# The order of SyncE's first loads and stores, and of GpSimd's first five steps, in a fused attention and two-layer kernel

## The reference

```python
q_d = q.reshape(B, H, Sd, 4, D).mean(axis=3)         # k_d, v_d likewise; Sd = 144
out_up = np.repeat(sm_attn(q_d, k_d, v_d), 4, axis=2)   # attention over pooled positions
mask = np.abs(pos[:, None] - pos[None, :]) < 4          # each position sees 7 neighbours
out_local = softmax(where(mask, scale * q @ k.T, -1e9)) @ v
x = (out_up + out_local)    # as 2304 tokens x 512
x = ((x @ w_a) * (x @ w_b)) @ w_out                     # 512 -> 1536 -> 512
h = x @ w_in                                            # 512 -> 1024
solu = h * softmax(h)
out = layernorm(solu) * g_ln @ w_out2                   # 1024 -> 512
```

## Time and profile before

| what | value |
|---|---|
| median of 3 runs | 793.23 us (791.5 to 793.58) |
| profiled execution, its own time | 793.58 us |
| its span, first to last instruction | 791.4 us |
| TensorE busy | 759.7 us, 96% of the span |
| TensorE busy from 0 to 160 us | 133.3 us |
| VectorE busy | 560.9 us, 71% |
| ScalarE, GpSimd busy | 298.2 us (38%), 214.7 us (27%) |
| DMA | 117.27 MB, 148 GB/s in the mean |
| TensorE's granted clock, mean | 0.998 of full speed |

### The profile page before, as it was taken

One profiled execution on the slowest core, in us unless ns is written; L12 is line 12 of the kernel. 1 busy time (PEld: TensorE's weight loads), 2 busy tenths in 40 slices (PEclk: granted clock), 3 DMA queues, 4 the chain that ended last, 5 costly groups with the idle time before them and its releaser, 6 DMA issues.

```text
span 791.4 us, 12269 instructions
## 1 busy us (share of the span) xinstructions
PE 759.7 (96%) x4440; PEld 695.3 (88%) x4440; DVE 560.9 (71%) x975; ACT 298.2 (38%) x819; POOL 214.7 (27%) x260
## 2 busy tenths in 40 slices
PE   6878889899999999999999999999999999999998
PEld 5767888799999999999999999999988888888886
DVE  4579999979979787778777876022467666666663
ACT  3443655454353525344524424224322212222222
POOL 2467977638414421041001111121100000000000
PEclk9999999999999999999999999999999999999999
DMA  9999958584887586683956433637121011011011
GB/s 189 192 237 221 217 117 258 199 259 149 265 244 243 169 244 183 186 203 106 256 163 188 149 107 110 205 102 228 39 66 54 27 54 54 27 55 53 27 41 41
DMA packets 96652, 117.27 MB, mean 148 GB/s; under 512 B 19921, under 2 KB 59603, under 8 KB 96593
## 3 DMA queue, kind: packets, MB, share of 16 engines
q1 hardware_dynamic: 81872, 106.98, 49.0%
q10 hardware_dynamic: 14721, 9.51, 4.2%
HBM read 95.62 MB, written 20.84 MB: 147 GB/s over the span
## 4 chain that ended last, share of the span: by engine, by line
PE 79%; DVE 0%; ACT 0%; issue 0%; DVEq 0%
PE psum L851 25%; PE psum L853 24%; PE psum L852 24%; PE psum L963 2%; PE psum L807 1%; PE psum L787 1%; PE psum L797 1%; PE psum L818 1%; PE psum L769 0%; DVE acc L1470 0%; DVE accT L1479 0%; ACT p_pool L1059 0%; ACT out_sb L1262 0%; ACT out_d L1077 0%; DVE ab_f L1381 0%
## 5 line engine op out<-in xcount | busy, mean ns | idle before, releaser
L851 PE MATMUL psum<-x_hi,w_hi 128*128 128x384 f32 x576 | 199.5, 346 | 2.3 <-DVE x_lo L1375 1.4
L853 PE MATMUL psum<-x_hi,w_lo 128*128 128x384 f32 x576 | 194.1, 337 | 0.0
L852 PE MATMUL psum<-x_lo,w_hi 128*128 128x384 f32 x576 | 193.9, 337 | 0.0
L851 PEld LDWEIGHTS psum<-x_hi,w_hi 128*128 128x128 f32 x576 | 109.2, 190 | 6.5 <-issue 4.6
L852 PEld LDWEIGHTS psum<-x_lo,w_hi 128*128 128x128 f32 x576 | 109.4, 190 | 0.0
L853 PEld LDWEIGHTS psum<-x_hi,w_lo 128*128 128x128 f32 x576 | 109.0, 189 | 0.0
L1381 DVE TENSOR_TENSOR ab_f<-psum,a_sb 128x384 f32<-128x384 f32 x72 | 39.8, 553 | 90.9 <-PE psum L853 62.0
L851 PE MATMUL psum<-ab_hi,wo_hi 128*128 128x384 f32 x288 | 99.8, 346 | 3.3 <-issue 3.3
L853 PE MATMUL psum<-ab_hi,wo_lo 128*128 128x384 f32 x288 | 96.6, 335 | 0.0
L852 PE MATMUL psum<-ab_lo,wo_hi 128*128 128x384 f32 x288 | 96.4, 335 | 0.0
L1689 POOL TENSOR_TENSOR raw<-raw 96x256 f32<-96x256 f32 x60 | 55.5, 951 | 123.2 <-DMA raw<-in_q 59.2
(11 more groups left out here) (147 smaller groups left out, 1420.0 us busy)
## 6 DMA issues: line engine op xcount, KB each, us to landing
wo_hi<-wo_hi_scratch SPq DMA_DIRECT2D x53, 256.0 KB, 2.7
wo_lo<-wo_lo_scratch SPq DMA_DIRECT2D x53, 256.0 KB, 3.1
k_u<-in_k SPq DMA_DIRECT2D x11, 576.0 KB
v_u<-in_v SPq DMA_DIRECT2D x11, 576.0 KB
k_u<-in_k SPq DMA_DIRECT2D x17, 288.0 KB
v_u<-in_v SPq DMA_DIRECT2D x17, 288.0 KB
wo_raw<-in_moe_w_out SPq DMA_DIRECT2D x19, 256.0 KB, 4.9
raw<-in_v SPq DMA_DIRECT2D x8, 576.0 KB, 6.7
```

Of the source, the lines that this page charges most:

```text
L851: mm(dst, wh, xh, start=first, stop=False, skip_group_check=not check)
L852: mm(dst, wh, xl, start=False, stop=False, skip_group_check=not check)
L853: last = mm(dst, wl, xh, start=False, stop=end, skip_group_check=not check)
```

## The change

Three things change. In SyncE's list for the head, the first block of w_out and the two stores of pooled v of batch 0 go ahead of the unit loads of q and k; the loads of w_out's second block and of weights 1 go ahead of raw (1, 2); the third block of w_out goes ahead of raw (1, 0); and the two stores of batch 1 go ahead of the wait for `x_summed` and of `load_weights(2)`. On GpSimd, `normalise(2)` goes between the two halves of the sums of pooled v. The two waits ahead of GpSimd's later sums are written as one expression: for tau 0 it still wants `x_lo_ready` at PPB = 4, and for tau 2 it now wants `hp_normed` at 4 where it wanted 2.

```diff
             load_weights(0)
+            load_wo(0)
+            store_vd(0, 0)
+            store_vd(0, 1)
             load_unit_q(1, 0)
             load_unit_k(1, 0)
-            store_vd(0, 0)
-            store_vd(0, 1)
             load_vd(0)
+            load_wo(1)
+            load_weights(1)
             load_raw(1, 2, 0)
             load_raw(1, 2, 1)
-            load_wo(0)
-            load_wo(1)
-            load_weights(1)
+            load_wo(2)
             load_raw(1, 0, 0)
             load_raw(1, 0, 1)
-            load_wo(2)
+            store_vd(1, 0)
+            store_vd(1, 1)
 
             sp.wait_ge(s.x_summed, PPB)
             load_weights(2)
-            store_vd(1, 0)
-            store_vd(1, 1)
...
             normalise(1)
             pool_rows(0, 2, 0)
+            normalise(2)
             pool_rows(0, 2, 1)
-            normalise(2)
             normalise(3)
             for tau in (2, 0):
 
-                if tau == 2:
-                    pool.wait_ge(s.hp_normed, 2)
-                else:
-                    pool.wait_ge(s.x_lo_ready, PPB)
+                pool.wait_ge(s.hp_normed if tau == 2 else s.x_lo_ready, PPB)
                 for half in range(2):
                     pool_rows(1, tau, half)
```

## The result

The changed kernel is slower: 800.35 us (median of 4 runs, 798.28 to 801.35) against 792.37 us for the kernel before (790.88 to 793.58), a ratio of 1.0098 [1.0069, 1.0127]. That is 8.0 us, four times the forecast of 2.0, and outside the range of 791 to 799.5 us. The execution that was profiled took 798.9 us with a span of 797.1, against 793.58 and 791.4: 5.3 and 5.7 us more.

What follows compares the result with a forecast made beforehand. It took TensorE, 96% of the span, as the bound, with v_d on the path at the head. Between +1.3 (GpSimd's burst) and +2.6 (v_d) it took +2.0: 793.58 + 2.0 = 795.6 us, median 795.5, range 791 to 799.5.

Steps and rivals of the forecast that it cites:

- the relief: Head: raw (1, 2) sums no longer overlap VectorE's last head steps, giving back 1.25 us, bounds 0 and 1.5.
- the lean to slower: Whole kernel: chance 0.45 that it measures slower, against 0.42 same and 0.13 faster.
- When v_d lands: Head: v_d, queued behind the unit loads, first used at 44.3 and not 41.72, so +2.6 us.
- The bytes are the same, and the hole in the DMA is only moved (32 to 35): DMA in the head: same traffic, its idle gap merely shifted to 32 to 35 us, at no cost.
- The rest at nothing: Other loads and stores SyncE issues in a different place or time: their readers have cover, so 0 us.
- Stores (1) land by 63: SyncE: batch 1's stores land by 63 us, so raw (1, 1) goes out near 65 as before.
- GpSimd's burst: First tile: sums from 52.0 to 66.7, then weight_low and wo_low to 71.6, setting the second gate, +1.3 us.
- The burst runs contended: Rival, GpSimd in the first tile: sums at contended lengths, +5.0 us, 798.5 us in all; chance 0.27.
- +1.3 here: First tile: end of GpSimd's sums and low parts at 71.6, 1.3 us later; lower end for the +2.0 taken.
- +2.6 of v_d: Head: lateness of v_d's first use without any relief; upper end for the +2.0 taken.
- everything that it loses is paid: Head: v_d is on the path with 1.77 us of wait, so any delay of it lengthens the kernel.
- the wait itself costs nothing: GpSimd: hp_normed at 4 is met by 51.35, before raw (1, 2) lands at 52, so 0 us.

Runs made afterwards that it cites:

- e3: Changed kernel with load_vd(0) moved ahead of the unit loads of q and k: 799.98 us, ratio 1.0079.
- e12: Kernel before with only load_wo(3) moved, to behind the first load_unit_v: 798.7 us, ratio 1.0072.
- e4: Changed kernel with the two stores of batch 1 back behind load_weights(2): 799.9 us, ratio 1.0083.
- e13: Changed kernel with load_vd(0) ahead of the unit loads, ten of twelve raw (1, 0) additions left out, load_wo(3) ahead of raw (1, 1): 797.66 us, 1.0044.
- e6: Changed kernel with ten of GpSimd's twelve additions for raw (1, 0) left out: 799.82 us, ratio 1.0083.
- e10: Changed kernel with load_wo(3) ahead of the loads of raw (1, 1), nothing left out: 801.33 us, ratio 1.0093.
- e7: Kernel before with ten of GpSimd's twelve additions for raw (1, 0) left out: 793.66 us, ratio 1.0009.
- e8: Kernel before with stores of batch 0, v_d, raw (1, 2) and raw (1, 0) issued ahead of unit loads, wo(1), weights(1): 794.0 us, 1.0019.
- e16: Kernel before with only load_wo(0) and the two stores of batch 0 ahead of the unit loads: 794.98 us, ratio 1.0015.
- e9: Changed kernel with ten of twelve raw (1, 0) additions left out and load_wo(3) ahead of raw (1, 1): 798.38 us, ratio 1.0059.
- e11: e8 with load_wo(3) ahead of raw (1, 1): 792.4 us, ratio 0.9986.
- e14: e11 with the unit load of v moved from n = 3 to n = 6: 793.52 us, ratio 1.0008.
- e15: Kernel before with load_wo(3) ahead of raw (1, 1) and the unit load of v at n = 6: 795.1 us, ratio 1.0022.
- e1: Kernel before with only GpSimd's part of the change: 795.6 us, ratio 1.0024.
- e2: Kernel before with only SyncE's part of the change: 797.35 us, ratio 1.0047.
- e5: Changed kernel with load_raw(1, 2) ahead of load_wo(1) and load_weights(1): 800.47 us, ratio 1.0102.

## Why the prediction was wrong

Right were the first steps on GpSimd and SyncE: `normalise(2)` at 28.70 (about 29 predicted), second sums to 33.0 (33.6), the unit loads at 33.40, `load_vd(0)` at 38.77 (39.2). Right was the relief: v_d is 4.9 us later and the first up product 3.6, so 1.3 us came back, as worked out; with GpSimd idle, `hp_den` took 0.16 us for both pairs and the normalisation 0.45. Right was that all of it lies before 160 us, and the lean to slower (0.45).

1. **"When v_d lands" was mis-sized.** I took 5.1 us from issue to use (39.2 to 44.3), bounds 43.3 to 46; it took 7.8 (38.77 to 46.60). I had let the unit loads run at 220 GB/s from 35.0, but the queue was empty when SyncE began to issue them, and the DMA share was 0.57 from 34 to 38 us, at 151 to 154 GB/s. The four loads of q alone carry 0.38 MB and took 2.65 us to issue, which is 148 GB/s. That v_d stands behind the unit loads is borne out: ahead of them, in e3, it took 4.9 us from issue to use (36.30 to 41.15). The 0.3 to 0.7 us that I allowed from the last byte to the waiting engine stand in no row; block 3 before landed at 78.17 and was read at 78.20. First product: +3.6, not +1.35.

2. **"The bytes are the same, and the hole in the DMA is only moved (32 to 35)" was false in its second half.** The bytes are the same (117.27 MB), but 6.3 us of DMA time are free around it instead of 2.3, and there is a second hole, 60 to 70 us, with 4.9 us. I had drawn the store's wait as a delay for v_d alone. It is one for everything behind it in SyncE's list, and the queue had been nearly full.

3. **"The rest at nothing" failed.** It said that weights(2) go out at some 59.5 and raw (1, 1) near 65 as today, because "Stores (1) land by 63". That rests on two quiet halves of sums from 52.0 on, to 59.3. In fact the first store waited for sums that ended at 59.5 and the second for sums that ended at 65.6. Real: weights(2) at 65.99, raw (1, 1) at 71.26, and wo(3), which I didn't list at all, at 72.39 instead of 66.77. The cover for weights(2) was enough; that of wo(3) was nothing, since ScalarE already waited 2.60 us for it before. e12 shows what a late wo(3) costs in the kernel before: 5 us. In the changed kernel it isn't a term to add, but a second bound on the same point: the block landed 1.1 us before ScalarE, held by the wait for `w_lo`, came to read it. And two things kept it back here: block 0's down product, which ended at 71.28 (in e4 that alone holds the load to 71.98), and SyncE's stand (in e3 and e13, with v_d early, that alone holds it to 74.27 and 71.50).

4. **The burst was mis-sized, and its path was wrong.** This is the step of the sum that failed most: GpSimd's burst was priced at +1.3 us. I put the new start at 52.0 (it was 55.06) and four halves at 3.67 us each, 14.7; they took 20.6, and the first `w_lo` behind them started at 75.62 instead of 66.7. The rival *The burst runs contended* had the sums near their size (18.5 us), but priced them at +5.0, so at 798.5, with a start 3 us too early. It was the better forecast and still 1.85 us short of the median. I had chosen the quiet length by a half that ran where VectorE had little to do. Of the four later ones before, the first took 3.4 us and the other three 5.3, 5.4 and 4.4 (partly in the earlier trace rows). As for the path: I had the burst hold a multiply of VectorE and, through it, the second gate. But the second gate came at 70.84, 0.3 us later than before, in the middle of the sums; what waited for their end was TensorE, 5.36 us, for the low part of block 2's weights, which I had put nowhere on the path.

5. **A sum over one path was the wrong form.** I took a mean between "+1.3 here" and "+2.6 of v_d" as if one path led through both. The runs show limits beside each other, ending within a few us: the burst, the `w_out` landings and v_d's chain. Take one away in the changed kernel and the time stays (e3, e6, e10: 1.0079 to 1.0093, against 1.0098); take one away in the kernel before, and it stays as well (e7: 1.0009, e8: 1.0019); delay the landing, and it is paid (e12: 1.0072). Of the three, v_d is the one of which it isn't shown that it costs anything by itself: in e16 its delay was gone by block 3. So the premise that "everything that it loses is paid" isn't borne out. In thirteen of the eighteen kernels (all but e9, e11, e13, e14 and e15) the first accumulator is turned 46.3 to 47.6 us after ScalarE reads block 3, whatever was changed ahead of it. In six of them (the kernel before, e3, e6, e7, e8 and e12) that read waits for the landing, in the other seven the profile names no wait for it, though in five of them (the changed kernel, e1, e2, e5 and e16) it had landed at most 1.1 us before. In the five other kernels it is 48.2 to 50.7 us, and there block 4 or 6 is waited for. The change delayed v_d, the burst and the landings, and that fits with no one undo giving it back.

For the rewritten wait, "the wait itself costs nothing" holds in the changed kernel (the load came at 55.06, and the last of the four normalisations had ended 1.5 us earlier, at 53.6) but not for the edit as such: with SyncE's old order (e1) it holds the sums from 43.97 to 48.50, and that half costs 0.24%.

What stays open: of the loss, 3.5 us remain with the three cuts together. The late block 4 and the late sums are seen there, but that they hold the rest is argued, not shown: SyncE's two stands weren't removed in one run with everything else. Nor did any run lengthen the burst alone by a known amount, as e12 did for the landing. The profiled executions differ by 5.7 us, the medians by 8.0; in the other 2 us I can't point to a place.

## What to carry to other kernels

A transfer that waits in an in-order list of issues can delay every landing behind it; list all of them with their readers' slack and with what else each of them waits for, not just the one that is known to be late, and ask whether the queue had ever been empty. Where several limits end within a few us of each other, removing one may show nothing, as here in either kernel: delay one by a known amount (e12) to see whether it counts, and cut them together to see what they hold. Price a burst of work at its contended rows when it will run beside a busy engine.

## What was unexpected of the hardware

Single VectorE instructions were held for whole stretches while GpSimd worked without gaps. VectorE's timeline after:

```profile
67.90 0.93 DVE L1385 TENSOR_TENSOR ab_lo<-ab_f,ab_hi 128x384 fp32r<-128x384 f32 x1
...
76.13 6.13 DVE L1385 TENSOR_TENSOR ab_lo<-ab_f,ab_hi 128x384 fp32r<-128x384 f32 x1
```

The same instruction took 0.93 us at 67.90 and 6.13 us at 76.13, over `w_lo` and `wo_lo` of GpSimd; before, another one was held for 5.14, mostly over the same two steps. Gapless work of GpSimd isn't enough for it: beside the sums, from 65.7 to 76 us after, no VectorE instruction took over 1.62 us. Which one is held, the runs don't show. GpSimd's steps took longer as well: four halves of sums took 20.6 us, 5.1 each, against 3.5 for the half at 29.55. And a store of 144 KB landed in 2.0 us with nothing queued ahead of it (the second store of batch 0 after), against 11.8 and 8.5 us before.
